# Only the diagonal blocks of L are written to DRAM, eight transfers per pair, and read back in one contiguous transfer

## The chip, the cores and the metric

The kernel runs on one core of a Trainium2 chip. The metric is the device time of one execution in microseconds. The profile is of one execution.

## The reference

A recurrent attention over 768 steps in 4 x 8 heads of width 40, then two feed-forward parts:

```
for t in range(S):
    y[:, :, t] = einsum('bhd,bhde->bhe', rt, state)
    Sa = einsum('bhde,bhe->bhd', state, at)
    state_decay = state * wt[:, :, None, :] - einsum('bhd,bhe->bhde', Sa, bt)
    state = state_decay + einsum('bhd,bhe->bhde', vt, kt)
```

The outputs of all heads are put side by side (3072 x 320) and go through `x @ w_in`, a softmax-weighted unit with a layer norm, `@ w_out`, and then through a second pair of weights with a leaky unit between them.

## The kernel before

The recurrence is worked in chunks of 64 steps. A group m (of 24) is one chunk of one half of the batch: 16 heads, eight in the lower and eight in the upper 64 partitions. Two neighbouring groups make a pair p (of 12). In each group TensorE makes for every head a 64 x 64 matrix L, which must be inverted (as a unit triangular matrix) to solve for the chunk's updates. The four 16 x 16 blocks on each diagonal are inverted first. For that a pair's 32 matrices have 128 diagonal blocks, and each of the 128 partitions (a lane) takes one of them.

The way to the lanes goes through DRAM. ScalarE copies L into the tile `lb` (`copy_l`). SP writes `lb` to the DRAM scratch `l_scr` (`l_write`, L204) in two transfers of 64 partitions, 256 KB each as the profile counts them, in runs of 256 bytes. The scratch gives each band of 16 rows one row of padding words more, so that a view with the right pitch finds the diagonal block of every lane at its start. `l_read` (L210) waits until both writes have landed (`l_out`) and reads the blocks into `s_in`, 16 runs of 64 bytes per lane. The solve runs on VectorE for pair 0 and on POOL for the others (`solve`, L814 and L816 its two operations), and leaves the inverse blocks and their transposes in `s_x`. `d_write` (L218) writes these to `d_scr` in runs of 1 KB, and `d_read` (L226) spreads them with eight transfers of 32 KB into `dd`, each for 16 partitions, in runs of 64 bytes. TensorE's `horner` (L341) uses them.

The order on SP is written out by hand. After the prologue, step n of 24 issues: load_a(n+7); in even steps l_read of pair (n+4)/2; load_wkb(n+8), load_v, save_y of the step before, load_rv; in odd steps d_write of pair (n+3)/2, which waits for POOL's solve, then l_write of pair (n+5)/2, then d_read of pair (n+3)/2, which waits until d_write has landed. In some steps a load of a feed-forward weight follows (L1034). Each queue is in order: an instruction behind a waiting one waits too. In the prologue l_write(0) stands between load_wkb(3) and load_a(4), l_write(1) ahead of d_write(0), and l_write(2) behind load_wkb(7), ahead of load_a(7). The reads of pair 0 are split, four on SP and four on ACT (`d_read` there, L715).

Other work that the text speaks of: POOL multiplies `a` in place (`scale_a`, L793), after which ACT copies it (`spread_a`, L709) for TensorE's scores (L310). VectorE runs the scan of w (L493) on the tile `wkb` of a group, at the end of the step before the one in which POOL needs it. SP's own operations are lines 178 (wkb), 185 (a), 207 (l_write), 215 (l_read), 223 (d_write) and 232 (d_read).

After the attention, TensorE works through the feed-forward parts, which begin beside the last attention steps.

Of the kernel before, what the change touches and what calls it, by code (L numbers as in the profile page):

```python
# [7 lines left out]
F32 = mybir.dt.float32  # L8
# [4 lines left out]
B, NH, SEQ, HD = 4, 8, 768, 40  # L13
T = 64
NC = SEQ // T
NG = NC * (B // 2)
HALF = 64
SB = 16
NB = T // SB
TP = T + 2  # L20
LANE = SB * T + SB
P = 128
DM = NH * HD
FF1, FF2 = 1024, 2048
# [16 lines left out]
def attention(nc, ctx, core, front, wkb_in, a_in, rv_in, v_in, masks_in, l_scr, d_scr, x_scr):  # L41
# [19 lines left out]
    def ring(name, count, shape):  # L61
        return [sb(f"{name}{i}", shape) for i in range(count)]
# [4 lines left out]
    lb = ring("lb", 3, [P, 2, NH, T])  # L67
# [22 lines left out]
    x = ring("x", 2, [P, NH, T])  # L90
    st_sum = sb("st_sum", [P, NH, HD])
    st = ring("st", 2, [P, NH, HD])
    s_in = [early_sb(f"s_in{i}", [P, SB, SB]) for i in range(2)]
# [21 lines left out]
    l_done, l_ready, ka_ready = sem("l_done"), sem("l_ready"), sem("ka_ready")  # L115
    kbn_done, kbn_ready = sem("kbn_done"), sem("kbn_ready")
    l_out, l_back, d_out, d_back = sems("l_out", 2), sems("l_back", 2), sems("d_out", 2), sems("d_back", 2)
# [9 lines left out]
    HR = [slice(0, HALF), slice(HALF, P)]  # L127
# [18 lines left out]
    def use(m, size, each):  # L146

        return (m // size + 1) * each
# [13 lines left out]
    def d_block(p, b):  # L162
# [2 lines left out]
        scr = d_scr[p].rearrange("k l x -> (k l) x").rearrange("(l b) (s t) -> b s l t", b=2 * NB, t=SB)  # L165
        return dd[p % 2][b * SB:b * SB + SB].rearrange("p k g h t -> p (k g h) t")[:, :, t:t + SB], scr[b]

    def sync(sp, beside):
        def load_wkb(m):
            wait(sp, kbn_done, 2 * (m - 2))  # L170
            if m in (1, 2):
                sp.wait_ge(wkb_set, 2 * m)
            if m == 0:
                sp.dma_start(w[m], wkb_in[m, :, 0:NH * TP]).then_inc(first_w_loaded, 16)
                sp.dma_start(wkb[m][:, NH * TP:], wkb_in[m, :, NH * TP:]).then_inc(wkb_loaded[m], 16)
            else:
                for h in range(2):
                    sp.dma_start(wkb[m % 3][ER[h]], wkb_in[m, ER[h]]).then_inc(wkb_loaded[m % 3], 16)

        def load_a(m):  # L180
            if m < 7:
                sp.wait_ge(al_set[m], 1)
            wait(sp, rhs_done, m - 6)
            for h in range(2):
                sp.dma_start(al[m % 7][ER[h], h].rearrange("p h t -> p (h t)"),
                             a_in[m, ER[h], h * NH * T:(h + 1) * NH * T]).then_inc(a_loaded[m % 7], 16)

        def load_v(m):
            if m < 3:
                sp.wait_ge(v_set, m + 1)  # L190
            wait(sp, st_done, m - 2)
            for h in range(2):
                sp.dma_start(sv[m % 3][HR[1 - h], h].rearrange("p h d -> p (h d)"),
                             v_in[m, h]).then_inc(v_loaded[m % 3], 16)

        def load_rv(m):
            if m < 3:
                sp.wait_ge(rvu_set, m + 1)
            wait(sp, y_done, m - 2)
            for h, planes in enumerate([slice(2, 4), slice(0, 2)]):  # L200
                sp.dma_start(rvu[m % 3][ER[h], :, planes].rearrange("p h k t -> p h (k t)"),
                             rv_in[m, h].rearrange("e (h x) -> e h x", h=NH)).then_inc(rvu_loaded[m % 3], 16)

        def l_write(p):  # L204
            sp.wait_ge(l_ready, 8 * p + 8)
            for h in range(2):
                sp.dma_start(l_scr[p, :, h, 0:T * T].rearrange("l (s t) -> s l t", t=T),
                             lb[p % 3][HR[h]].rearrange("p g h t -> p (g h) t")).then_inc(l_out[p % 2], 16)

        def l_read(p):  # L210
            wait(sp, first_solve, SOLVE if p > 1 else 0)
            wait(sp, solve_step, (p - 2) * SOLVE)
            sp.wait_ge(l_out[p % 2], use(p, 2, 32))
            lanes = l_scr[p].rearrange("l f x -> (l f x)").rearrange("(l x) -> l x", x=LANE)
            sp.dma_start(s_in[p % 2][:], lanes[:, 0:SB * T].rearrange("l (s t) -> l s t", t=T)[:, :, 0:SB])\
              .then_inc(l_back[p % 2], 16)

        def d_write(p):  # L218
            if p == 0:
                sp.wait_ge(first_solve, SOLVE)  # L220
            else:
                sp.wait_ge(solve_step, p * SOLVE)
            sp.dma_start(d_scr[p].rearrange("k l x -> l k x"),
                         s_x[:].rearrange("p k s t -> p k (s t)")).then_inc(d_out[p % 2], 16)

        def d_read(p, blocks=range(2 * NB)):  # L226
            if p < 2:
                sp.wait_ge(dd_set, p + 1)
            wait(sp, x_taken, 4 * (2 * p - 2))
            sp.wait_ge(d_out[p % 2], use(p, 2, 16))  # L230
            for b in blocks:
                sp.dma_start(*d_block(p, b)).then_inc(d_back[p % 2], 16)  # L232

        def save_y(m):
            sp.wait_ge(y_stored, m + 1)
            sp.dma_start(x_scr[m], x[m % 2][:].rearrange("p n t -> p (n t)")).then_inc(y_saved[m % 2], 16)

        def prologue():
            load_wkb(0)
            load_a(0)  # L240
            load_wkb(1)
            load_a(1)
            sp.dma_start(masks[:], masks_in).then_inc(masks_loaded, 16)
            load_wkb(2)
            load_a(2)
            load_a(3)
            load_wkb(3)
            l_write(0)
            load_a(4)
            l_read(0)  # L250
            load_wkb(4)
            for m in range(2):
                load_v(m)
                load_rv(m)
            l_write(1)
            d_write(0)
            d_read(0, range(0, 2 * NB, 2))
            l_read(1)
            load_a(5)
            load_wkb(5)  # L260
            load_a(6)
            load_wkb(6)
            d_write(1)
            d_read(1)
            load_wkb(7)
            l_write(2)

        def step(n):
            if n + 7 < NG:
                load_a(n + 7)  # L270
            if n % 2 == 0 and n + 4 < NG:
                l_read((n + 4) // 2)
            if n + 8 < NG:
                load_wkb(n + 8)
            if n + 2 < NG:
                load_v(n + 2)
            if n > 0:
                save_y(n - 1)
            if n + 2 < NG:
                load_rv(n + 2)  # L280
            if n % 2 == 1:
                if n + 3 < NG:
                    d_write((n + 3) // 2)
                if n + 5 < NG:
                    l_write((n + 5) // 2)
                if n + 3 < NG:
                    d_read((n + 3) // 2)

        prologue()
        for n in range(NG):  # L290
            step(n)
            beside(sp, n)
        save_y(NG - 1)
# [372 lines left out]
    def scalar(act, beside):  # L666
        def copy_l(m, piece):

            act.wait_ge(l_done, 2 * m + 1 + piece)
            wait(act, x_done, 4 * (m - 6) + 1)  # L670
            src = score_banks(m)[:, piece * 512:piece * 512 + 512].rearrange("p (n a t) -> p n a t", n=4, a=2)
            for half in range(2):
                own = HR[half]
                if m >= AHEAD:
                    wait(act, ka_ready, half * (4 * m + 2 * piece + 1))
                act.copy(lb[m // 2 % 3][own, m % 2, piece * 4:piece * 4 + 4], src[own, :, half]).then_inc(l_ready, 1)  # L676
# [25 lines left out]
        def spread_a(m):  # L702
# [5 lines left out]
            for half in range(2):  # L708
                act.copy(a_bd[ER[half], half], al[m % 7][ER[half], half]).then_inc(a_bd_ready, 1)  # L709

        def d_read(p, blocks):
            act.wait_ge(dd_set, p + 1)
            act.wait_ge(d_out[p % 2], use(p, 2, 16))
            for b in blocks:
                act.dma_start(*d_block(p, b)).then_inc(d_back[p % 2], 16)  # L715
# [16 lines left out]
        def prologue():  # L732
            act.wait_ge(a_bd_set, 1)
            act.copy(pu[:], a_bd[:, 0].rearrange("p h t -> p (h t)")).then_inc(psum_set, 1)
            act.copy(py[:], a_bd[:, 0].rearrange("p h t -> p (h t)")).then_inc(psum_set, 1)
            act.wait_ge(psum_set, 2)
            spread_a(0)
            for m in range(AHEAD - 2):
                if m == 0:
                    spread_a(1)  # L740
                copy_l(m, 0)
                copy_l(m, 1)
                if 0 < m < AHEAD - 3:
                    spread_a(m + 1)
                take_kbn(m)
            d_read(0, range(1, 2 * NB, 2))
            spread_a(AHEAD - 2)
            copy_l(AHEAD - 2, 0)
            copy_l(AHEAD - 2, 1)
            take_rhs(0)  # L750
            take_kbn(AHEAD - 2)
# [877 lines left out]
```

## Time and profile before

| | |
|---|---|
| Median of three runs | 991.1 us (987.02 to 992.26) |
| Profiled execution, time | 993.74 us |
| its span, granted clock | 992.0 us, 0.974 |
| PE busy | 913.4 us, 92% |
| DVE, ACT, POOL busy | 656.3, 435.2, 244.2 us |
| DMA queue q1 | 154588 packets, 65.54 MB |
| HBM read, written | 45.98 MB, 19.66 MB |

The span runs from the first to the last instruction that the profiler recorded; the execution's own time is 1.74 us longer. Busy time is the time in which an engine had work; PE is TensorE's matmul side, PEld its weight loads, DVE VectorE, ACT ScalarE, POOL GpSimd. SPq and ACTq are the instruction queues of SyncE and ScalarE, which issue DMAs; these are not counted as busy. The attention fills roughly the first 430 us, the rest is feed-forward.

### The profile page before, as it was taken

Reading aid. Unit: us, or ns where it says so; the run is one execution under the profiler, and the core shown is the slowest. Engines: PE = TensorE matmul, PEld = TensorE weight load, DVE = VectorE, ACT = ScalarE, POOL = GpSimd, SP = SyncE. Lnnn points to the kernel's source line nnn. Section 1 sums busy time; section 2 is a strip of 40 time slices with the busy share of each in tenths; the row PEclk is TensorE's granted clock in tenths of the full one; section 3 lists DMA queues with packets and bytes.
Section 4 is the critical chain, followed back from the end, with each engine's and each line's share of the span. In section 5 each row is a group of like instructions: output and inputs, shape, how many; then the busy total and the mean of one; then the engine's idle time right before and its main releaser. Section 6 shows DMA issues by size and latency. Waiting matters only on the chain.

```text
span 992.0 us, 31301 instructions
## 1 busy us (share of the span) xinstructions
PE 913.4 (92%) x13248; PEld 871.0 (88%) x13248; DVE 656.3 (66%) x1135; ACT 435.2 (44%) x892; POOL 244.2 (25%) x453
## 2 busy tenths in 40 slices
PE   3388999998999989888999999999999999999997
PEld 3377899988998988777999999999999999999997
DVE  7957878878777665567565657575756656565734
ACT  3234544544445534246353535353444435353523
POOL 8675555766556550000000000000000000000000
PEclk9679999999999999799999999999999999999999
DMA  5726666657667544252001010000000000000000
GB/s 158 126 68 153 140 125 137 153 140 169 128 141 163 128 84 110 63 178 63 11 17 28 1 28 1 27 0 26 0 26 0 26 13 13 26 0 13 2 14 14
DMA packets 156813, 67.32 MB, mean 68 GB/s; under 512 B 120172, under 2 KB 146412, under 8 KB 156700
## 3 DMA queue, kind: packets, MB, share of 16 engines
q1 hardware_dynamic: 154588, 65.54, 28.0%
q8 instruction: 89, 1.46, 0.6%
q10 hardware_dynamic: 2112, 0.13, 0.2%
q14 instruction: 24, 0.20, 0.1%
HBM read 45.98 MB, written 19.66 MB: 66 GB/s over the span
## 4 chain that ended last, share of the span: by engine, by line
PE 52%; POOL 15%; DVE 9%; DMA 8%; issue 7%; SPq 6%; ACT 3%; ACTq 0%; POOLq 0%; DVEq 0%
PE acc L1095 6%; POOL s_t L814 6%; POOL s_x L816 5%; SPq L232 5%; PE acc L1096 5%; PE acc L1097 5%; PE mid L1095 4%; PE mid L1096 4%; PE mid L1097 4%; PE bank L1095 3%; PE bank L1097 3%; PE bank L1096 3%; DMA d_scr<-s_x 3%; DMA al<-a_features_first 2%; PE bank L1128 2%
## 5 line engine op out<-in xcount | busy, mean ns | idle before, releaser
L1354 POOL TENSOR_TENSOR stats<-stats 128x1 f32<-128x1 f32 x24 | 13.2, 549 | 549.0 <-DVE stats L1416 549.0
L1441 DVE SCALAR_TENSOR_TENSOR stage<-mid,slopes 128x512 f32<-128x512 f32 x96 | 66.3, 691 | 106.2 <-ACT slopes L1282 106.2
L1095 PE MATMUL acc<-wo_h,act_h 128*128 128x320 f32 x384 | 121.9, 317 | 8.4 <-DVE act_l L1368 7.7
L1278 ACT ACTIVATE stage<-mid 128x512 f32<-128x512 f32 x96 | 57.1, 594 | 160.2 <-PE mid L1166 160.2
L1096 PE MATMUL acc<-wo_h,act_l 128*128 128x320 f32 x384 | 118.9, 310 | 0.0
L1097 PE MATMUL acc<-wo_l,act_h 128*128 128x320 f32 x384 | 118.5, 309 | 0.0
L1095 PE MATMUL mid<-zT_h,w_h 128*128 128x256 f32 x384 | 107.7, 281 | 2.4 <-DVE zT_l L1368 2.4
L1096 PE MATMUL mid<-zT_h,w_l 128*128 128x256 f32 x384 | 107.4, 280 | 0.0
L1097 PE MATMUL mid<-zT_l,w_h 128*128 128x256 f32 x384 | 107.1, 279 | 0.0
L793 POOL TENSOR_TENSOR al<-al,prod 40x512 f32<-40x512 f32 x48 | 70.5, 1469 | 97.3 <-DMA al<-a_features_first 84.9
L1282 ACT ACTIVATE slopes<-stage,minus_alpha 128x256 f32<-128x256 f32 x192 | 87.3, 502 | 3.1
L1095 PEld LDWEIGHTS acc<-wo_h,act_h 128*128 128x128 f32 x384 | 72.4, 188 | 13.2 <-issue 11.2
L1095 PEld LDWEIGHTS mid<-zT_h,w_h 128*128 128x128 f32 x384 | 72.5, 189 | 3.6 <-DVE zT_l L1368 2.8
L1096 PEld LDWEIGHTS mid<-zT_h,w_l 128*128 128x128 f32 x384 | 72.6, 189 | 0.8
L1097 PEld LDWEIGHTS mid<-zT_l,w_h 128*128 128x128 f32 x384 | 72.7, 189 | 0.0
L1096 PEld LDWEIGHTS acc<-wo_h,act_l 128*128 128x128 f32 x384 | 72.5, 189 | 0.0
L1097 PEld LDWEIGHTS acc<-wo_l,act_h 128*128 128x128 f32 x384 | 72.5, 189 | 0.0
L1368 DVE TENSOR_TENSOR act_l<-stage,act_h 128x512 fp32r<-128x512 f32 x96 | 66.5, 692 | 3.3
L310 PE MATMUL pa<-a_bd,wkb 128*128 128x128 f32 x336 | 47.5, 302 | 19.5 <-DMA masks<-masks_in 11.2
L676 ACT COPY lb<-pa 64x256 f32<-64x256 f32 x84 | 30.8, 366 | 76.2 <-PE pa L310 45.4
L814 POOL TENSOR_TENSOR s_t<-s_in,s_x 128x15 f32<-128x15 f32 (+4 forms) x165 | 59.7, 362 | 12.9
L310 PEld LDWEIGHTS pa<-a_bd,wkb 128*128 128x128 f32 x336 | 44.8, 215 | 20.3 <-DMA masks<-masks_in 11.2
(162 smaller groups left out, 2405.7 us busy)
## 6 DMA issues: line engine op xcount, KB each, us to landing
wkb<-wkb_features_first SPq DMA_DIRECT2D x46, 242.5 KB
rvu<-rv_features_first SPq DMA_DIRECT2D x48, 160.0 KB
l_scr<-lb SPq DMA_DIRECT2D x24, 256.0 KB, 4.4
x_scr<-x SPq DMA_DIRECT2D x24, 256.0 KB, 4.6
al<-a_features_first SPq DMA_DIRECT2D x48, 80.0 KB
sv<-v_time_first SPq DMA_DIRECT2D x48, 80.0 KB, 4.7
out<-y_sb SPq DMA_DIRECT2D x12, 320.0 KB, 2.2
d_scr<-s_x SPq DMA_DIRECT2D x12, 256.0 KB, 2.3
```

What stands on the lines that cost most here:

```text
L232: sp.dma_start(*d_block(p, b)).then_inc(d_back[p % 2], 16)
L310: ins = pe.matmul(banks[:, h * P:(h + 1) * P], kbT[m % 3][:, h].rearrange("p a b -> p (a b)"), a_bd[:, :, h], start=True, stop=True)
L793: pool.tensor_tensor(al[m % 7][r, half], al[m % 7][r, half], prod[m % 9][r, :, 0:T], ALU.mult)\
L814: link(pool.tensor_tensor(s_t[:, 0:n_t, 0:n_j], coef, row, ALU.mult))
L816: link(pool.tensor_tensor(tgt, tgt, s_t[:, 0:n_t, 0:n_j], ALU.subtract))
L1095: pe.matmul(o, left[0], right[0], start=start, stop=False)
L1096: pe.matmul(o, left[1], right[0], start=False, stop=False)
L1097: return pe.matmul(o, left[0], right[1], start=False, stop=stop)
L1278: act.activation(neg[q % 2][:], mid[q % 2][:], ACT.Relu, scale=-1.0).then_inc(neg_ready, 1)
L1282: act.activation(slope[q % 2][:, cols], neg[q % 2][:, cols], ACT.Copy, scale=minus_alpha[:, 2 * q + f:2 * q + f + 1]).then_inc(slope_ready, 1)
L1368: return dve.tensor_tensor(out_, in_, hi.bitcast(F32), ALU.subtract)
L1441: dve.scalar_tensor_tensor(out=act_f[q % 2][:], in0=mid[q % 2][:], scalar=0.0, in1=slope[q % 2][:], op0=ALU.max, op1=ALU.add).then_inc(act ...
```

## The change

`l_scr` shrinks to (12 pairs, 16 head lanes, 8 blocks, 256 words): 1 KB for each lane's block, without gaps. `l_write` issues eight transfers, one for each block place b: 16 partitions of `lb`, of which only 16 of the 64 columns of every head are taken, in runs of 64 bytes; 16 KB of data each. `l_read` waits for eight landings and reads 1 KB per lane, contiguous on both sides. For pair 0 SP issues the even four of the eight and ACT the odd four, between its copies of group 1 and its spread of `a`.

```
-LANE = SB * T + SB
...
+    def l_block(p, b):
+
+        t = (b % NB) * SB
+        rows = lb[p % 3][b * SB:b * SB + SB].rearrange("p g h t -> p (g h) t")[:, :, t:t + SB]
+        return l_scr[p, :, b].rearrange("l (s t) -> s l t", t=SB), rows
...
-        def l_write(p):
+        def l_write(p, blocks=range(2 * NB)):
             sp.wait_ge(l_ready, 8 * p + 8)
-            for h in range(2):
-                sp.dma_start(l_scr[p, :, h, 0:T * T].rearrange("l (s t) -> s l t", t=T),
-                             lb[p % 3][HR[h]].rearrange("p g h t -> p (g h) t")).then_inc(l_out[p % 2], 16)
+            for b in blocks:
+                sp.dma_start(*l_block(p, b)).then_inc(l_out[p % 2], 16)
 
         def l_read(p):
...
-            sp.wait_ge(l_out[p % 2], use(p, 2, 32))
-            lanes = l_scr[p].rearrange("l f x -> (l f x)").rearrange("(l x) -> l x", x=LANE)
-            sp.dma_start(s_in[p % 2][:], lanes[:, 0:SB * T].rearrange("l (s t) -> l s t", t=T)[:, :, 0:SB])\
-              .then_inc(l_back[p % 2], 16)
+            sp.wait_ge(l_out[p % 2], use(p, 2, 128))
+            sp.dma_start(s_in[p % 2][:].rearrange("l s t -> l (s t)"),
+                         l_scr[p].rearrange("l b x -> (l b) x")).then_inc(l_back[p % 2], 16)
...
-            l_write(0)
+            l_write(0, range(0, 2 * NB, 2))
...
+        def l_write(p, blocks):
+            act.wait_ge(l_ready, 8 * p + 8)
+            for b in blocks:
+                act.dma_start(*l_block(p, b)).then_inc(l_out[p % 2], 16)
...
                 copy_l(m, 0)
                 copy_l(m, 1)
+                if m == 1:
+                    l_write(0, range(1, 2 * NB, 2))
...
-    l_scr = nc.dram_tensor("l_scr", (NC, 2 * NH, 2, NB * LANE), F32, kind="Internal").ap()
+    l_scr = nc.dram_tensor("l_scr", (NC, 2 * NH, 2 * NB, SB * SB), F32, kind="Internal").ap()
```

## Rows read from the trace of the kernel before

**Rows 1.** The page's chain that ended last, shares of the span.

```profile
PE 52%; POOL 15%; DVE 9%; DMA 8%; issue 7%; SPq 6%; ACT 3%; ACTq 0%; POOLq 0%; DVEq 0%
```

**Rows 2.** Table of stretches: stretch, its length, busy us and instructions, clock, DMA share, GB/s.

```profile
100.20:342.90 242.70, 230.69 (x6268) 218.64 (x6260) 192.52 (x308) 116.00 (x259) 147.33 (x288) 1.00 0.64 143
```

**Rows 3.** PE's waits: total us, times, longest us.

```profile
PE px L341 <- DMA dd<-d_scr: 13.8, 1, 13.8
PE px L341 <- issue: 4.2, 5, 1.6
```

**Rows 4.** Timeline of SP's queue, first and last of nine pairs: start, us, instruction.

```profile
100.20 0.39 SPq L223 DMA_DIRECT2D d_scr<-s_x  x1
100.64 2.36 SPq L207 DMA_DIRECT2D l_scr<-lb  x2
103.48 6.65 SPq L232 DMA_DIRECT2D dd<-d_scr  x8
...
342.88 0.38 SPq L223 DMA_DIRECT2D d_scr<-s_x  x1
343.30 1.43 SPq L207 DMA_DIRECT2D l_scr<-lb  x2
345.20 6.65 SPq L232 DMA_DIRECT2D dd<-d_scr  x8
```

**Rows 5.** Timelines: SP's load_wkb of two even groups and VectorE's scans on them.

```profile
201.98 3.16 SPq L178 DMA_DIRECT2D wkb<-wkb_features_first  x2
...
209.92 1.30 DVE L493 TENSOR_TENSOR_SCAN prod<-wkb,seeds 128x528 f32<-128x528 f32 x1 [0.40 <-DMA wkb<-wkb_features_first]
...
233.00 1.85 SPq L178 DMA_DIRECT2D wkb<-wkb_features_first  x2
...
240.41 1.29 DVE L493 TENSOR_TENSOR_SCAN prod<-wkb,seeds 128x528 f32<-128x528 f32 x1
```

**Rows 6.** Timelines: ACT's copy of `a` and PE's scores on it, group 14.

```profile
195.33 1.26 ACT L709 COPY a_bd<-al 40x512 f32<-40x512 f32 x2 [1.18 <-POOL al L793]
...
200.16 1.95 PE L310 MATMUL pa<-a_bd,wkb 128*128 128x128 f32 x16
```

**Rows 7.** Timeline of SP's queue: d_read of pair 1.

```profile
68.89 4.02 SPq L232 DMA_DIRECT2D dd<-d_scr  x8
```

**Rows 8.** Table of stretches: behind an l_write, and with d_reads alone.

```profile
103.20:106.20 3.00, 3.00 (x109) 2.93 (x104) 2.97 (x3) 2.77 (x5) 0.47 (x1) 1.00 0.92 170
...
71.00:74.00 3.00, 2.32 (x18) 1.94 (x16) 1.53 (x3) 1.35 (x4) 0.30 (x1) 1.00 0.64 63
```

**Rows 9.** Chain of waits from 38 to 52 us: start, us, what.

```profile
40.63 2.17 DMA d_scr<-s_x
...
44.40 4.58 DMA dd<-d_scr
...
49.02 1.98 PE px L341 x32
```

**Rows 10.** DMA issues by tile: count, KB each, median us from issue to landing.

```profile
dd<-d_scr SPq DMA_DIRECT2D x92, 32.0 KB, 3.0
...
s_in<-l_scr SPq DMA_DIRECT2D x12, 128.0 KB, 3.6
```

**Rows 11.** Timeline of SP's queue in the prologue.

```profile
35.13 1.37 SPq L207 DMA_DIRECT2D l_scr<-lb  x2
...
44.85 0.49 SPq L215 DMA_DIRECT2D s_in<-l_scr  x1
...
74.14 1.30 SPq L207 DMA_DIRECT2D l_scr<-lb  x2
...
75.48 3.28 SPq L185 DMA_DIRECT2D al<-a_features_first  x2
```

**Rows 12.** Timeline of ACT in the prologue, idle time before in brackets.

```profile
23.52 1.26 ACT L709 COPY a_bd<-al 40x512 f32<-40x512 f32 x2 [3.45 <-POOL al L793]
...
48.77 1.26 ACT L709 COPY a_bd<-al 40x512 f32<-40x512 f32 x2 [12.88 <-POOL al L793]
```

## The prediction

> **What bounds the kernel now.** The chain of waits comes first. On the page it gives PE 52% of the span and POOL 15%, SPq 6% [rows 1]: the reader is to see that between 85 and 370 us it runs round a loop of the attention part: the solve of a pair on POOL, d_write, d_read, load_a and load_wkb on SP, the scaling of `a` on POOL, the next solve. The table of stretches is there to doubt that. Between the third pair's d_write (100.2 us) and the eleventh's (342.9) PE is busy 230.69 of 242.7 us at clock 1.00, POOL 147.33 [rows 2]. The list of waits settles it: PE waited for the inverse blocks `dd` once, for 13.8 us, and never again; the largest of its short attention waits is 4.2 us in all [rows 3]. So TensorE's own work sets the pace, and the loop runs beside it at about the same period: d_write follows d_write after (342.88 - 100.20) / 8 = 30.3 us [rows 4]. The question is how much slack the loop has, since the change lengthens SP's part of it.
>
> Two rows give the slack. SP issues load_wkb of the even groups right behind the d_reads and the l_read. In one pair the issue ended at 201.98 + 3.16 = 205.14 and VectorE's scan, which had waited 0.40 us for it, began at 209.92: 4.8 us from the end of the issue to use. In the next pair the issue ended at 234.85 and the scan began at 240.41, 5.6 us later, without a wait [rows 5]. So the slack here is 0 to 0.8 us. For `a` it is larger: the copy that waited for POOL ended at 195.33 + 1.26 = 196.59, and PE's matmuls on it began at 200.16, 3.6 us later [rows 6].
>
> **The steady pairs (nine, p = 2 to 10).** Behind each d_write stands l_write of the next pair, then eight d_reads. Now l_write is 2 transfers, 2.36 us in the first such pair and 1.43 us in the last; the d_reads took 6.65 us in both [rows 4]. From the start of d_write to the end of the d_reads that is 9.93 us in the first (110.13 - 100.20) and 8.97 us in the last; the nine have a mean of 8.73 us. Where no l_write stands in front, the same eight d_reads take 4.02 us [rows 7], so 1.8 us on the mean of 5.8 us is a stall, and I put it down to the 2 x 256 KB of l_write still passing: in that stretch the DMA share is 0.92 at 170 GB/s, in one with d_reads alone 0.64 at 63 GB/s [rows 8].
>
> After: 8 l_write transfers of 16 KB in 64-byte runs. No such row exists; the nearest is the d_read, the same shape in the other direction with twice the runs: 4.02 / 8 = 0.50 us each [rows 7]. I take that: 0.46 (to the end of d_write) + 8 x 0.50 + 0.04 + 4.02 = 8.5 us, against 8.73: -0.2 us per pair, so long as the stall goes with the bytes. The d_out wait (d_write lands in 2.2 us, rows 9) vanishes under the 4.0 us. Bounds of one transfer: 0.39 us (the d_write row) and 0.70 us (1.43 / 2, an l_write now, rows 4), plus the gap of 0.04: 3.4 to 5.9 us for eight, so -0.6 to +1.9 us beside my value; if the stall stays, another +1.8. Against now, per pair: -0.8 to +3.5 us.
>
> The runs' size: `l_write` keeps its 2048 runs per pair, each of 64 instead of 256 bytes. Were each run as dear as now, 512 KB at 170 GB/s are 3.1 us [rows 8], still less than the 4.0 us over which they are now issued; so they don't pile up unless a run of 64 bytes costs more than 1.3 times one of 256. The Trainium skill (DMA: Bandwidth & Descriptors, Specifications) speaks against the change here: under 512 bytes a transfer is not at line rate, because the DMA engine does a read-modify-write. Its Rules for kernel authors add that under 64 KB per transfer one pays mostly overhead, and the page's anatomy of one DMA (of the path through GpSimd) gives 2.0 us of fixed cost; six more in a row would be, as an estimate, 12 us per pair. The trace has eight 32 KB transfers issued in 4.02 us, so such overheads overlap here; that small writes to DRAM cost no more than small reads no row shows.
>
> The read back: 2048 runs of 64 bytes become 128 of 1 KB, contiguous. s_in lands in 3.6 us now; a 256 KB write of 1 KB runs lands in 2.17 us [rows 9]. I take 1.2 us less, between 0 and 1.4. It is issued just ahead of load_wkb, so the even load_wkb lands up to 1.2 us sooner: slack of the loop 0 to 0.8 becomes about 1 to 2. Since PE paces, what the loop gains is not passed on; only the scan's 0.40 us wait goes: -0.4 us.
>
> **The start.** PE's one long wait ends at 49.02 us on the inverse blocks of pair 0, four reads on ACT and four on SP. ACT's last, issued at 44.40, took 4.58 us to land [rows 9], while the median of such reads is 3.0 [rows 10]; SP's l_read(1), 2048 runs, is issued at 44.85 beside it [rows 11]. With 128 runs I let the blocks land about 1.5 us sooner. But the next matmuls need a copy of `a` that ACT ends at 48.77 + 1.26 = 50.03 [rows 12] and now start at 51.00, when the first product ends: -1.0 us is all that can be had; it may be 0. It is kept, because the solve of pair 1 waits for that same l_read.
>
> l_write(0) is split. ACT's four issues (4 x 0.50 = 2.0 us) come after its copies of group 1; ACT then sat idle 3.45 us before 23.52, waiting for POOL [rows 12]. The cover is 1.4 us larger than the need: 0. Behind them on ACT stand only that copy and PE's third group. l_write(1) starts at 35.13; eight issues end at 39.2, and d_write(0) is due at 40.63 [rows 9, 11]: 0, or +0.2 at 0.70 us each. l_write(2) starts at 74.14; its 4.0 us end at 78.2 where the two of now end at 75.44, but load_a behind them then stalled for 3.28 us [rows 11]. Unstalled (0.73 us) it ends at 78.9 against 78.76. l_read(2), which waits for the last of the eight to land, is issued some 1 us later than now and lands 1.2 us faster: 0.
>
> **The sum**, against the profiled execution of 993.74 us (span 992.0 and 1.74 around it): -1.0 - 0.4 = -1.4, so 992.3. The profiled execution lies 2.6 us above the median of the runs, 991.1; so about 989.7 us. The feed-forward part is untouched and starts as much earlier as the attention ends.
>
> **Rivals.**
> (a) SP becomes the bound (slower). Place: SP's queue between d_write and load_wkb in each of nine pairs. The extra issues cost their time and the stall stays, since 2048 runs are still in front of the d_reads. Price with the stall alone: +1.6 per pair, 14.4, less the slack of about 2 us, gives +12: 1002 us; with 0.70 us issues as well +3.5 per pair: 31.5 - 2 = +29.5, 1019 us. It decides from a lengthening of 2 / 9 = 0.2 us per pair, which is why it has much weight. For it: d_reads sit behind the same number of runs. Against: the stalled d_reads coincide with a DMA share of 0.92, and the new runs come spread over 4 us. If each run of 64 bytes cost twice one of 256 (6.2 us for 2048 of them, not 3.1), the d_reads would wait 2.2 us per pair for them: +18, 1008 us; I give that 0.05 of the 0.26. That is what the Trainium skill's read-modify-write (above) could do here. If the eight passed one behind the other at 3.0 us each [rows 10], it would be 20 us per pair; the eight d_reads in 4.02 us exclude it to 0.01. That is the Trainium skill's overhead rule (above).
> (b) More comes than I allow (faster). PE's short waits, such as the 4.2 us in all before px [rows 3], are up to 12.0 us of 242.7 not busy [rows 2]; if they come from late loads and late VectorE, 4.7 MB less traffic closes most of them: -9, some 981 us. Against: DVE waited for loads only 0.4 us there.
> (c) Nothing at all (same): the transfers were hidden, the first wait is limited by other reads, 991.1.
>
> **How the numbers follow.** Chances: forecast 0.47, (c) 0.13, (a) 0.26, (b) 0.14. The likeliest has its own range of 987 to 994. What a measurement of this kernel can tell from no change is about 0.5%, 5 us: 986.1 to 996.1. (a) goes to slower but for 0.01; (b) to faster but for 0.01, and 0.05 of the forecast lies below 986.1. Faster 0.18, same 0.57, slower 0.25. The range reaches into (b) and, further, into (a): 984 to 1003.
>
> **What would show it.** Right: the eight l_write issues of a steady pair take about 4 us, the d_reads behind them about 4 and not 5.8; s_in lands in about 2.4 us; PE's long wait ends near 48 us; the time between d_writes stays at 30.3; the packets of q1 fall from 154,588 by some 12 x (2048 - 128) = 23,000 and the bytes written by 4.7 MB. Wrong: l_write issues of 0.7 us, d_reads still near 6 us, scans that wait for wkb in many pairs, a period above 30.6. It would fall altogether if the period moved though SP's stretch did not.

## The result, and the profile after

The change makes the kernel slower: a median of 1006.2 us (1000.9 to 1009.9, four runs) against 991.7 us (987.0 to 1000.2, four runs), a ratio of 1.0119 with a 95% interval of 1.0077 to 1.0160. (The ratios here are worked out from all fast runs and not from the two medians, which alone would give 1.0146.) On another occasion the pair gave 1.0091 (1.0052 to 1.0130). The forecast was 989.7 us, with 1003 as the upper end of its range. The profiled execution took 1003.92 us, its span is 1002.1 us: 10.1 us more than before.

The bytes went where they were expected to go. From the page of the kernel after, the DMA queues and the traffic in HBM:

```profile
q1 hardware_dynamic: 131612, 60.76, 24.3%
...
HBM read 45.98 MB, written 14.94 MB: 61 GB/s over the span
```

Written bytes fell by 4.72 MB, q1's packets by 22,976. The time was lost on SP's queue. Its timeline for the first and the last of the nine steady pairs, after (start, us, instruction):

```profile
98.36 0.39 SPq L226 DMA_DIRECT2D d_scr<-s_x  x1
98.80 5.35 SPq L212 DMA_DIRECT2D l_scr<-lb  x8
104.25 4.10 SPq L235 DMA_DIRECT2D dd<-d_scr  x8
...
356.80 0.39 SPq L226 DMA_DIRECT2D d_scr<-s_x  x1
357.24 5.89 SPq L212 DMA_DIRECT2D l_scr<-lb  x8
363.23 4.96 SPq L235 DMA_DIRECT2D dd<-d_scr  x8
```

Beside [rows 4] the reader is to see two things. The writes take 5.35 and 5.89 us where they took 2.36 and 1.43. The d_reads take 4.10 and 4.96 where they took 6.65: most of the stall behind the large writes is gone. The second is smaller than the first. Over the nine pairs the end of the d_reads lies 10.64 us behind the start of d_write, against 8.73 before, +1.9 us. And d_write now follows d_write after (356.80 - 98.36) / 8 = 32.3 us, against 30.3: +2.0 us. The loss lies there. At the third pair's d_write the kernel after is 1.8 us ahead (98.36 against 100.20), at the eleventh's 13.9 us behind (356.80 against 342.88); of these 10.1 us are left at the end of the span.

How it reaches TensorE is seen behind the third of the nine d_writes (163.28 us). Timelines of SP, PE and VectorE (idle time before an instruction, and what ended it, in brackets):

```profile
175.49 0.73 SPq L183 DMA_DIRECT2D wkb<-wkb_features_first  x2
...
176.31 1.15 PE L344 MATMUL px<-dd,lb 64*64 64x64 f32 x32 [1.22 <-DMA dd<-d_scr]
...
182.75 1.26 DVE L496 TENSOR_TENSOR_SCAN prod<-wkb,seeds 128x528 f32<-128x528 f32 x1 [7.24 <-DMA wkb<-wkb_features_first]
...
184.79 1.97 PE L344 MATMUL px<-dd,lower 64*64 64x64 f32 x32 [4.78 <-DVE lower L556]
```

Everything that stands behind the scan on VectorE waits for the late wkb, `lower` among it, and PE for that. Before, such a scan waited once in this part, for 0.40 us [rows 5]. The list of waits from 85 to 390 us, after (total us, times, longest):

```profile
PE px L344 <- DVE lower L556: 15.8, 9, 4.8
...
PE px L344 <- DMA dd<-d_scr: 1.6, 3, 1.2
...
DVE prod L496 <- DMA wkb<-wkb_features_first: 18.0, 3, 7.2
```

The three waits of VectorE stand before the three long gaps of PE, of 4.78, 3.77 and 4.27 us (ending at 184.79, 250.55 and 315.83 us): the loop slips against TensorE for a pair or two unseen, then comes a gap of some 4 to 5 us.

### The profile page after: what moved, and what is told of

The parts are those of the page before. It is cut to its first block, busy times and chain, and to the rows that moved or that the text cites. A ratio compares the mean times of both kernels' runs of the same rounds, so it can differ in the third digit from the quotient of the medians.

```text
span 1002.1 us, 31373 instructions
## 1 busy us (share of the span) xinstructions
PE 917.3 (92%) x13248; PEld 874.9 (87%) x13248; DVE 656.1 (65%) x1135; ACT 435.6 (43%) x892; POOL 239.1 (24%) x453
## 4 chain that ended last, share of the span: by engine, by line
PE 50%; POOL 15%; SPq 11%; DVE 8%; issue 7%; DMA 6%; ACT 3%; POOLq 0%; DVEq 0%; ACTq 0%
PE acc L1105 6%; POOL s_x L826 5%; POOL s_t L824 5%; PE acc L1106 5%; PE acc L1107 5%; SPq L212 5%; SPq L235 5%; PE mid L1105 4%; PE mid L1106 4%; PE mid L1107 4%; PE bank L1105 3%; PE bank L1107 3%; PE bank L1106 3%; DMA s_in<-l_scr 2%; PE bank L1138 2%
## 5 line engine op out<-in xcount | busy, mean ns | idle before, releaser
L803 POOL TENSOR_TENSOR al<-al,prod 40x512 f32<-40x512 f32 x48 | 68.0, 1417 | 114.8 <-DMA al<-a_features_first 102.4
L826 POOL TENSOR_TENSOR s_x<-s_x,s_t 128x15 f32<-128x15 f32 (+4 forms) x165 | 59.5, 361 | 12.9
```

The costliest lines, as they stand in the source:

```text
L803: pool.tensor_tensor(al[m % 7][r, half], al[m % 7][r, half], prod[m % 9][r, :, 0:T], ALU.mult)\
L826: link(pool.tensor_tensor(tgt, tgt, s_t[:, 0:n_t, 0:n_j], ALU.subtract))
```

## The experiments

All ratios are to the kernel before, run on the same chip. The three columns on the right are from the profiled executions, in us: from the start of d_write to the first d_read and to the end of the eight, both as means of the nine pairs, and the period, (eleventh d_write - third) / 8. They are of one execution each, and where it lay among the runs differs: that of e10 took 984.7 us with a median of 991.4, that of e11 981.6 with 986.6.

| Kernel | Ratio, 95% interval | d_reads begin | end | period |
|---|---|---|---|---|
| before | | 2.67 | 8.73 | 30.3 |
| after | 1.0119 (1.0077, 1.0160) | 5.81 | 10.64 | 32.3 |
| e5_after_again | 1.0091 (1.0052, 1.0130) | 5.88 | 10.59 | 32.2 |
| e1_half_act | 0.9999 (0.9964, 1.0034) | 3.11 | 8.27 | 30.4 |
| e2_before_plus6 | 1.0325 (1.0243, 1.0407) | 7.56 | 12.47 | 34.1 |
| e3_read_in_runs | 1.0135 (1.0075, 1.0194) | 5.68 | 10.65 | 32.3 |
| e4_wkb_first | 1.0111 (1.0045, 1.0178) | 5.31 | 10.17 | 31.8 |
| e8_lwrite_first | 0.9990 (0.9957, 1.0023) | 3.13 | 7.70 | 30.9 |
| e6_quad | 0.9945 (0.9911, 0.9978) | 3.33 | 8.60 | 30.2 |
| e7_quad_half_act | 0.9911 (0.9873, 0.9949) | 2.92 | 7.84 | 29.8 |
| e9_a_first | 0.9973 (0.9940, 1.0006) | 6.89 | 11.68 | 30.2 |
| e10_before_a_first | 0.9968 (0.9927, 1.0010) | 4.64 | 9.81 | 29.9 |
| e11_quad_half_a_first | 0.9933 (0.9903, 0.9963) | 3.36 | 8.52 | 28.7 |
| e12_before_half_act | 0.9974 (0.9941, 1.0006) | 2.50 | 8.00 | 29.8 |

**e1: half of the writes on ScalarE.**

```
# SP, odd step
-                    l_write((n + 5) // 2)
+                    l_write((n + 5) // 2, range(0, 2 * NB, 2))
# ACT, behind take_uT(n)
+            if n % 2 == 0 and 0 < n and n + 4 < NG:
+                l_write((n + 4) // 2, range(1, 2 * NB, 2))
```

> The changed kernel with ScalarE issuing four of the eight writes of every pair from 3 on, behind its copies of the solution in the following step, where it otherwise waits for GpSimd; SP issues the other four. Theory Q (SP's queue between d_write and load_wkb is too long, by the time of issuing): from the start of d_write to the first d_read falls from 5.8 us to about 2.8 us, to the end of the d_reads from 10.6 to about 7.5, less than the 8.7 of the kernel before; the period falls from 32.3 to about 30, the stalls of VectorE on wkb vanish, and the time is 987 to 993 us. Theory M (the writes of 64 bytes or the larger number of transfers load the DMA engines, whoever issues them): the d_reads stay as late in landing, the time stays near 1003 to 1008 us. Theory P (GpSimd's solve is slowed by VectorE, since the two are out of step): solve times still vary between 13 and 18 us and the time stays above 1000 us.

Measured: 994.0 us against 994.1, the whole loss is gone; above the range that theory Q gave by 1 us, as the end of the d_reads came to 8.27 and not 7.5. VectorE's waits on wkb fell from 18.0 to 5.5 us and didn't vanish. SP's timeline of one pair:

```profile
223.21 0.41 SPq L226 DMA_DIRECT2D d_scr<-s_x  x1
223.66 2.07 SPq L212 DMA_DIRECT2D l_scr<-lb  x4
225.84 4.86 SPq L235 DMA_DIRECT2D dd<-d_scr  x8
```

The same eight transfers with the same bytes are still made, so neither their number nor their 64-byte runs cost anything that can be told from noise (0.9964 to 1.0034) when four of them aren't issued in this place. The d_reads begin 2.7 us sooner and take 5.16 us on the mean, not 4.83. One solve still took 17.1 us (the others 13.6 to 15.6), so theory P has no hold.

**e2: the kernel before with six small transfers more.**

```
+            for b in range(6):
+                t = (b % NB) * SB
+                sp.dma_start(l_more[p, :, b].rearrange("l (s t) -> s l t", t=SB),
+                             lb[p % 3][b * SB:b * SB + SB]...[:, :, t:t + SB]).then_inc(l_out[p % 2], 16)
# l_read waits for their landing too
```

> The kernel before with six more transfers behind the two of l_write: blocks 0 to 5 of L once more, 16 KB each in runs of 64 bytes, to a scratch that nobody reads, for every pair; the read in runs stays. Theory Q: the six cost about 6 x 0.55 us of SP's time in each pair, so the d_reads start 5.9 instead of 2.7 us behind d_write, and unlike in the changed kernel the 512 KB are still written, though earlier than the d_reads, so that these take 4 to 5 us; the time rises to 1005 to 1015 us. Theory M: as the bytes are the larger ones of before plus some, the same or more. If the smaller bytes of the changed kernel were what costs, and not the issues, the time would stay within 3 us of the kernel before.

Measured: 1025.0 us against 994.1, +31, which is Q's direction but beyond its range. SP's timeline:

```profile
207.34 0.41 SPq L228 DMA_DIRECT2D d_scr<-s_x  x1
207.80 2.77 SPq L207 DMA_DIRECT2D l_scr<-lb  x2
210.62 4.35 SPq L211 DMA_DIRECT2D l_more<-lb  x6
215.08 4.66 SPq L237 DMA_DIRECT2D dd<-d_scr  x8
```

The six alone take 4.35 us here, 0.73 each: the stall of the large writes falls on them now and the d_reads keep another part of it. The stretch grew by 12.47 - 8.73 = 3.7 us, the period by 3.8. As in the change itself, the period grew by what the stretch grew by. The profiled executions lie 32.9 us apart: 4.6 of it arise up to the third d_write (104.82 for 100.20), 30.3 in the eight periods behind it, and 2.0 are made good later. There was hardly any slack. The wait through which the loop passes this on is POOL's for load_a. From 85 to 390 us, before, after and here:

```profile
POOL al L793 <- DMA al<-a_features_first: 73.4, 8, 10.4
```

```profile
POOL al L803 <- DMA al<-a_features_first: 92.0, 8, 14.1
```

```profile
POOL al L798 <- DMA al<-a_features_first: 123.2, 9, 15.8
```

The solve that starts next stands behind this scaling on POOL, and the next d_write behind that solve.

**e3: the write part alone.**

```
-        return l_scr[p, :, b].rearrange("l (s t) -> s l t", t=SB), rows
+        return l_scr[p, :, b].rearrange("l (s t) -> s l t", t=2 * SB)[:, :, 0:SB], rows
# and in l_read
+            sp.dma_start(s_in[p % 2][:], l_scr[p].rearrange("l b (s t) -> (l b) s t", t=2 * SB)[:, :, 0:SB])
```

> The changed kernel with the scratch stretched so that each row of 16 words stands 128 bytes from the next: the eight writes as in the changed kernel, the read again in 16 runs of 64 bytes per lane. So the write part of the change without the read part. If the contiguous read brings the even load_wkb about 1 us sooner (as forecast), this is slower than the changed kernel by up to 1 us per pair, since the loop over SP now paces: 1006 to 1015 us. If the read's form is worth nothing, it is within 3 us of the changed kernel's 1006.

Measured: 1005.3 us (1.0135), not told apart from the contiguous read (1.0119 and 1.0091). Transfers to landing (median, last column), first the kernel after, then this one:

```profile
s_in<-l_scr SPq DMA_DIRECT2D x12, 128.0 KB, 3.1
```

```profile
s_in<-l_scr SPq DMA_DIRECT2D x12, 128.0 KB, 4.0
```

The contiguous read lands 0.9 us sooner and the time doesn't show it: the next solve waits for `a` first, and its scaling on POOL covers the read.

The read does more than land sooner. SP's issues of it and of load_wkb behind it, after and then here:

```profile
109.30 0.36 SPq L218 DMA_DIRECT2D s_in<-l_scr  x1
109.70 0.73 SPq L183 DMA_DIRECT2D wkb<-wkb_features_first  x2
```

```profile
111.67 0.59 SPq L218 DMA_DIRECT2D s_in<-l_scr  x1
112.30 2.26 SPq L183 DMA_DIRECT2D wkb<-wkb_features_first  x2
```

In the seven pairs that have such a load, its issue takes 0.72 to 0.74 us behind the contiguous read, 1.54 to 2.91 behind the 2048 short runs, and 1.55 to 3.16 in the kernel before. So the issue of wkb ends 13.3 us behind d_write in the kernel after and 14.9 here (12.6 before), yet the period is 32.3 in both. How late wkb is issued behind d_write doesn't set the period. load_a stands ahead of the read and gets nothing from it.

**e4: load_wkb of the even groups ahead of d_write.**

```
-            if n + 8 < NG:
+            if n + 8 < NG and (n % 2 == 1 or n == 0):
                 load_wkb(n + 8)
...
             if n % 2 == 1:
+                if n + 9 < NG:
+                    load_wkb(n + 9)
```

> The changed kernel with load_wkb of the even groups issued in the odd step before, ahead of d_write instead of behind the d_reads. Theory W (the late wkb, for which VectorE waits in order, is what TensorE feels of SP's lengthening): VectorE's waits on wkb vanish and so do TensorE's gaps of 4 to 5 us before px; the loop of solve and SP is still longer than TensorE's two steps, though, by 1 to 1.5 us per pair, against a slack of 4 to 7 us in the inverse blocks and in a: most is given back, 992 to 998 us. If the blocks or a are as late as wkb, TensorE waits for them instead in nearly every pair, and the time stays at 1002 to 1008 us.

Measured: 1004.0 us. The waits on wkb are gone, as theory W said, the time is not. Waits, 85 to 390 us, of DVE and of PE:

```profile
DVE prod L498 <- DMA wkb<-wkb_features_first: 0.2, 1, 0.2
```

```profile
PE pa L315 <- issue: 9.4, 6, 2.7
PE px L346 <- DMA dd<-d_scr: 8.4, 6, 2.7
```

PE now waits six times for the inverse blocks, and six times at the scores that need `a`. ACT, which copies `a` for them, waits for POOL's scaling 15 times (before the move 6 times, 19.0 us):

```profile
ACT a_bd L714 <- POOL al L805: 59.6, 15, 6.1
```

The move isn't pure: ahead of d_write, load_wkb makes SP wait for TensorE to free the tile (30.5 us in seven waits), though nine of these d_writes still waited for the solve after that. So wkb was only the first of three products of one late loop. Where one is taken away the next is due.

**e5, e8: the kernel after again, and with the writes moved ahead of d_write.** (The order of e8 in an odd step:)

```
                 if n + 5 < NG:
                     l_write((n + 5) // 2)
                 if n + 3 < NG:
                     d_write((n + 3) // 2)
```

> The changed kernel itself, so that the others are compared with it on one chip: 1.010 to 1.015 times the kernel before by every theory.

> The changed kernel with the eight writes of a pair issued on SP ahead of d_write instead of behind it (from pair 3 on): same transfers, same bytes, same queue, only moved into the 6 to 8 us in which SP sits waiting for the solve. Theory Q (SP's time between d_write and load_wkb, and nothing else): from d_write to the first d_read 2.3 us, to the end of the d_reads 6.5 to 7 us, solve to solve 29 to 30 us where the writes end before the solve does; if L is ready late, d_write comes up to 2 us late and about half is lost. Time 990 to 997 us. Theory M (number or size of transfers loads the DMA engines): 1003 to 1008 us.

Measured: 1007.0 us and 996.3 us, with 996.5 before. The ratio of e5, 1.0091, is just below the 1.010 that was expected. In e8 it is the same transfers, same bytes, same queue; only what they delay is different, and the time is that of the kernel before. It is not free: SP now waits for L, and d_write behind it, so that the period is 30.9 and not the 29 to 30 expected. SP's waits in the whole run:

```profile
SPq L212 <- ACT lb L679: 47.7, 11, 7.2
```

**e6, e7: four squares instead of eight blocks.**

```
-        t = (b % NB) * SB
-        rows = lb[p % 3][b * SB:b * SB + SB].rearrange("p g h t -> p (g h) t")[:, :, t:t + SB]
-        return l_scr[p, :, b].rearrange("l (s t) -> s l t", t=SB), rows
+        t = (b % 2) * 2 * SB
+        rows = lb[p % 3][b * 2 * SB:b * 2 * SB + 2 * SB].rearrange("p g h t -> p (g h) t")[:, :, t:t + 2 * SB]
+        return l_scr[p, :, b, 0:4 * SB * SB].rearrange("l (s t) -> s l t", t=2 * SB), rows
# l_scr: (NC, 2 * NH, NB, 2 * LANE), LANE = 2 * SB * SB + SB; l_read takes 16 runs of 64 bytes at that pitch
# e7: also half of the four on ACT, as in e1
```

> The changed kernel with four writes per pair instead of eight: squares of 32 x 32 words, each with two diagonal blocks, runs of 128 bytes, 256 KB per pair (before: 512, after: 128), read again in runs of 64 bytes through a padded pitch. Theory Q: four issues of 0.55 us end 2.7 us behind the start of d_write, about when it has landed, so that the d_reads start as early as in the kernel before; they take 4.8 us as the stall is smaller with half the bytes. End of d_reads at 7.6 us, against 8.7 before and 10.6 after. Time 0.997 to 1.001 of the kernel before, as TensorE paces there. If each 0.1 us of the loop counted even below the kernel before (the loop paces there too), 0.988 to 0.992. Theory M: half way, 1.006.

> The same four squares, two of them issued by ScalarE in the step after, so that SP's part is shorter still: end of the d_reads 6.8 to 7.3 us behind d_write, about 1.5 us less than before. If TensorE paces the kernel before, as forecast, nothing comes of it: 0.996 to 1.001. If the loop paces there, -1.5 us for each of nine pairs: 0.984 to 0.988.

Measured: 991.6 and 988.4 us against 996.5, both faster than the kernel before. Neither reading had this right: more than nothing, less than 1.5 us for each of nine pairs. The d_reads ended at 8.60 and 7.84 us, later than the 7.6 and the 6.8 to 7.3 that were expected. SP's timeline of a pair of e7:

```profile
218.59 0.40 SPq L228 DMA_DIRECT2D d_scr<-s_x  x1
219.04 1.43 SPq L213 DMA_DIRECT2D l_scr<-lb  x2
221.07 4.89 SPq L237 DMA_DIRECT2D dd<-d_scr  x8
```

The writes now fit under the landing of d_write, but the d_reads still take 4.9 us.

**e9, e10, e11: load_a ahead of the d_reads, in three kernels.**

```
-            if n + 7 < NG:
+            if n + 7 < NG and (n % 2 == 1 or n == 0):
                 load_a(n + 7)
...
             if n % 2 == 1:
...
+                if n + 8 < NG:
+                    load_a(n + 8)
                 if n + 3 < NG:
                     d_read((n + 3) // 2)
```

> The changed kernel with load_a of the even groups (the one that the next solve waits for) issued ahead of the eight d_reads instead of behind them; the eight writes stay where they are. Theory Q+L (the loop of solve, d_write, SP's issues, load_a, scaling and next solve paces the attention, in the kernel before as well): the next solve then waits only for l_read, which stays behind the d_reads; it starts some 14 us behind d_write instead of 17.1, the period falls by 2 to 3 us to about TensorE's own, and the time is 988 to 994 us, 0.990 to 0.998 of the kernel before, although all that the change added is still there. If the writes cost through the inverse blocks or wkb coming late, it stays at 1.005 to 1.010.

> The kernel before with the same move of load_a. By the forecast's reading (TensorE paces the kernel before, the loop has slack) nothing: 0.998 to 1.002. By theory Q+L the loop paced there too, at 30.3 us, and TensorE alone could do 29 or less: 0.985 to 0.993.

> The four squares, two of them on ScalarE, and load_a ahead of the d_reads: the shortest loop. With the loop well out of the way TensorE paces, so this and the kernel before with load_a moved should come out within 0.5% of each other, at 0.984 to 0.990; if the loop still paced, this is faster than both by 1 us per pair: 0.975 to 0.980.

Measured: 991.2, 991.4 and 986.6 us against 994.7. e9 has every transfer of the change, in the place where the change put it, and is as fast as e10 without them: 0.9973 and 0.9968. SP's timeline of a pair of e9:

```profile
221.72 0.40 SPq L226 DMA_DIRECT2D d_scr<-s_x  x1
222.18 5.71 SPq L212 DMA_DIRECT2D l_scr<-lb  x8
227.93 0.75 SPq L190 DMA_DIRECT2D al<-a_features_first  x2
228.78 5.28 SPq L235 DMA_DIRECT2D dd<-d_scr  x8
```

The d_reads end even later than in the kernel after, 11.7 us behind d_write, yet the next solve starts 15.6 us behind it instead of 17.1, and the period is back at 30.2. VectorE still waits for wkb, five times, but never for long (85 to 390 us; after, 18.0 us with one wait of 7.2):

```profile
DVE prod L498 <- DMA wkb<-wkb_features_first: 9.3, 5, 3.9
```

This is the test that closes the case: it is the way over load_a to the next solve on which the writes cost, not the inverse blocks and not the wkb as such. e10's 0.9968 is below 1 by less than theory Q+L wanted, and its interval reaches 1. e11's 0.9933 is within 0.5% of e10, as expected, but above its range of 0.984 to 0.990.

**e12: the kernel before with one of its two large writes on ScalarE.** (The second `dma_start` of l_write goes to ACT, at the place of e1.)

> The kernel before, its 512 KB in two transfers, with the second issued by ScalarE in the step after. It separates the bytes from the issues: SP's part loses 0.7 us of issue, hidden under the landing of d_write (2.3 us) in most pairs, so by issues alone 0.3 us per pair; the stall of the d_reads, 1.8 us, stays if the 512 KB cause it, and the time is 0.996 to 1.000. If the four squares with two on ScalarE (0.991) gained by the placing on ScalarE rather than by the bytes, this is at 0.991 too.

Measured: 992.4 us, 0.9974. The d_reads took 5.50 us, nearer to the 6.06 of before than to the 4.02 without writes [rows 7]. Its interval just overlaps that of e7, so whether e7 owes its lead to the bytes or to chance stays open.

## Why the prediction was wrong

Rival (a) came true in the main: SP's queue behind d_write became the bound, though the link that counts is load_a and not load_wkb. It was given 0.26 and a price of 1002 us for the case in which the stall stays, 1.6 us per pair; the median is 1006. Its sum came out otherwise: less than half of the stall stayed, and the issues cost the rest.

**The steps that failed.** First, the sum of a steady pair, 8.5 us, measured 10.64. Its two terms were both taken from the quickest row: 8 x 0.50 for the writes and 4.02 for the d_reads without a stall. The line of l_write in the kernel after, over all 92 issues on SP (min, median, max in ns):

```profile
L212 SPq DMA_DIRECT2D l_scr<-lb x92: 310/450/1703, 20.1 to 362.7; - x92
```

The median of 0.45 us is below what I took, but of the 72 in the nine pairs twelve take 1.09 us or more, one or two in every set of eight, so that the first d_read starts 5.8 us behind d_write and not 4.5. The d_reads take 4.83 us on the mean, so their stall fell from 2.0 to 0.8 us; I let it vanish. (Before, their mean was 6.06 us, not the 5.8 that I had worked out.) Both errors point the same way: +1.3 for the writes, +0.8 for the d_reads.

I had said that stall and bytes go together, and that fits more than half of it: the stall fell by 1.2 us of 2.0 with a quarter of the bytes and the same number of runs. The stretch of the eight writes and the one that answers to [rows 8], after:

```profile
98.80:104.10 5.30, 5.30 (x174) 5.07 (x174) 5.17 (x6) 4.09 (x8) 2.81 (x2) 1.00 0.40 74
103.20:106.20 3.00, 3.00 (x101) 2.85 (x97) 2.94 (x6) 0.61 (x1) 0.00 (x0) 1.00 0.23 23
```

The DMA engines are at 0.40 on the mean while eight issues take 5.35 us (0.28 to 0.43 in the other eight sets), at 0.23 where they were at 0.92. So the remaining stalls come with DMA engines that are mostly idle. What they are, and whether the 64-byte runs have a part in them, no run shows.

Second, the slack, and where I looked for it. I read 0 to 0.8 us at wkb, where the loop hands a product to TensorE, and hoped for 1.2 more from the contiguous read. The read landed 0.5 us sooner than before and not 1.2 (3.1 us for 3.6 [rows 10]) and freed about 1.3 us of SP's time behind it; e3 shows no gain from either in the time, and the waits for wkb, of which I let 0.40 us go, grew to 18.0. Neither touches the way that closes the loop: d_write, l_write, d_reads, load_a, the scaling, the next solve. The trace of the kernel before had that way without slack: in eight pairs POOL sat waiting for load_a (73.4 us, shown at e2), which SP issued right behind the d_reads. That there is next to no slack was right for all that: the loop passed its 1.9 us on whole (8 x 1.9 = 15.2 from the third to the eleventh d_write, 15.8 measured). What I should have done with it: a forecast of "-0.2 us per pair" that stands 0.4 us from the point where the sign turns is no forecast of no change.

Third, "TensorE's own work sets the pace". It didn't. PE was busy 230.69 of 242.7 us [rows 2], but e11 brings the same pairs in 229.4 us. Stretches of e11 and, below, of the kernel after (columns as in [rows 2]):

```profile
98.40:327.80 229.40, 226.04 (x6173) 215.21 (x6172) 185.12 (x303) 114.69 (x255) 141.28 (x288) 1.00 0.64 141
```

```profile
98.40:356.80 258.40, 237.75 (x6282) 225.18 (x6281) 193.10 (x310) 116.65 (x259) 144.46 (x288) 0.97 0.51 122
```

So in the kernel before the loop, at 30.3 us, was the longer of the two by up to 1.6 us: TensorE's work for two groups fits into 28.7. A PE that is busy for 95% of 30.3 us leaves 1.5 us of each, and about that much e11 took. The chain of waits on the page, which I set aside for the busy table, ran over this loop and was the better guide.

**What held.** The wait on d_out, which went (SP waited for it ten times from 85 to 390 us before, once after); ScalarE's four writes in its idle time at no cost, since its copy still began after an idle time of 3.45 us, at 23.50 for 23.52; the packets and the bytes. A 16 KB write in runs of 64 bytes lands in 1.9 us at the median, and in e1, with all of these writes, no cost of them shows in the time. The Trainium skill (DMA: Bandwidth & Descriptors, Specifications) has a read-modify-write under 512 bytes; no run here shows its cost by itself, nor rules out that it is part of the stalls that remain. With the same page's Rules for kernel authors, that transfers under 64 KB are mostly overhead, the trace agrees in so far as the overhead is SP's: 5.35 and 5.89 us for 128 KB, where 512 KB took 2.36 and 1.43 [rows 4].

**The start** was 1.8 us shorter up to the third d_write, where I had given 1.0, but not as I had it. PE's first products began at 48.71 us, only 0.3 earlier than at 49.02:

```profile
48.71 1.97 PE L344 MATMUL px<-dd,lb 64*64 64x64 f32 x32 [12.18 <-DMA dd<-d_scr]
```

From 49 to 62 us TensorE's granted clock was 0.80, before it was 0.63, and the next solution step came 2.2 us sooner (61.31 for 63.55). The loads did come earlier, and by the form of the read: behind l_read(1) the two issues of load_a take 0.73 us in the kernel after and in e1, e4, e5, e8 and e9, which all read contiguously, but 2.70 before and 2.73 in e3. But the 1.8 us may be scatter: e7 and e12 read in short runs and have their third d_write at 98.79 and 99.01 us, e1 reads contiguously and has it at 99.82.

## What to carry to other kernels

Where a loop runs through an in-order DMA queue, count the issues that stand between its wait and its next link, at the mean of the rows with their stalls and not at the quickest, and look whether the loop has any idle time of its own. That its period equals that of the busiest engine doesn't tell which of the two binds; here POOL's wait for load_a in nearly every pair did, and e11 with its period of 28.7 us. Measure the slack on the way that closes the loop, not where it hands a product to the busy engine. Bytes saved count there only by the stall that they take from the issues behind them (1.2 us a pair here). An issue moved off that stretch is worth up to its own time, whether it goes to another engine's idle time (e1), ahead of the wait (e8), or behind the link that the loop needs, by moving that link forward (load_a in e9). Here four writes of 32 x 32 words, two of them on ScalarE, gave 0.9911 (0.9873 to 0.9949), the best ratio; with load_a ahead of the d_reads besides, 0.9933 (0.9903 to 0.9963), not told apart from it.

## What the hardware showed that I had not expected

A gap of 4 to 5 us cost TensorE more than the gap. Stretches of the kernel after around the gap at 184.79 us, PE alone (length, busy, clock, DMA share, GB/s):

```profile
170.00:180.00 10.00, 8.78 (x294) 1.00 0.66 136
...
184.80:188.00 3.20, 3.20 (x38) 0.50 0.75 205
188.00:190.00 2.00, 2.00 (x11) 0.50 0.66 185
190.00:194.00 4.00, 4.00 (x95) 0.92 0.23 52
```

After the idle 4.78 us the granted clock was 0.50, the lower of its two levels (1.2 of 2.4 GHz), for the next 5 us, and the same products took longer. Sixteen of them one step earlier, at clock 1.00, and behind the gap:

```profile
165.19 2.05 PE L405 MATMUL pq<-rvu 128*128 128x128 f32 x16
...
186.69 3.78 PE L405 MATMUL pq<-rvu 128*128 128x128 f32 x16
```

From the end of one group's `pu` to the next that step took 23.2 us (175.1 to 198.3); the waits of 1.22 and 4.78 us explain 6.0 of the 8.8 us over the 14.4 of the step before, the clock the rest. The other two long gaps were followed by the same: the sixteen products took 3.44 and 3.66 us. Over the eight periods the mean clock was 0.97 where it had been 1.00, and of the 15.7 us by which they grew, 7.1 are busy time of PE (237.75 for 230.69) and 8.6 idle time. In the kernel before, PE's longest wait of this part was 1.6 us.

A read in many short runs held up the issue behind it. Two issues of load_wkb behind 128 runs of 1 KB took 0.73 us, behind 2048 runs of 64 bytes 2.2 us on the mean of seven (e3).

The last: an issue of l_write on SP that mostly takes 0.45 us took 1.09 to 1.70 us twelve times in 72, at least once in every set of eight, with the DMA engines at 0.28 to 0.43 on the mean.
